# An attention block and two feed-forward layers on one core: the first tile in halves, another order of loads, narrow tiles placed last, one lower part on its own

## The reference

```
scores = cap * tanh(q @ k.T / sqrt(64) / cap)          # 2 batches x 12 heads, 448 tokens, head size 64
attn   = exp(scores - max) / (sum(exp) + 1e-9)
x      = attn @ v                                       # 896 tokens x 768
h      = x @ w_in;  h = max(0.01 * h, h);  y = h @ w_out  # 768 -> 2048 -> 768
yn     = y / rms(y) * rms_g
out    = (silu(yn @ w_gate) * (yn @ w_val)) @ w_out2    # 768 -> 1536 -> 768
```

## Time and profile before

| what | before |
|---|---|
| median of 3 runs | 561.96 us (561.7 to 564.47) |
| the profiled execution's own time | 560.67 us |
| its span, first to last instruction | 558.9 us |
| PE busy | 553.1 us, 99% |
| DVE, POOL, ACT busy | 429.7, 323.6, 290.0 us |

### The profile page before, as it was taken

The page is one execution under the profiler, slowest core; times in us unless marked ns, Lnnn a source line. Parts: engine busy times, 40 slices in busy tenths (PEclk is TensorE's granted clock), DMA queues, the critical chain, the costliest instruction groups (busy, mean ns, idle before and its releaser), DMA issues.

```text
span 558.9 us, 7933 instructions
## 1 busy us (share of the span) xinstructions
PE 553.1 (99%) x2679; PEld 466.1 (83%) x2679; DVE 429.7 (77%) x594; ACT 290.0 (52%) x503; POOL 323.6 (58%) x282
## 2 busy tenths in 40 slices
PE   8999999999999999999999999999999999999997
PEld 5545554699999999999999999999999999999896
DVE  4459988695677799932159498999999999999963
ACT  6888889326445497431155355444434446824330
POOL 1025365478666653594383576766776896634672
PEclk9999999999999999999999999999999999999999
DMA  6254442123111112213022011122211111210521
GB/s 174 70 177 149 135 133 52 37 72 110 62 56 57 57 57 66 86 38 114 1 62 90 0 58 56 58 65 86 77 56 57 57 57 57 62 52 1 154 91 67
DMA packets 30007, 41.49 MB, mean 74 GB/s; under 512 B 17040, under 2 KB 19088, under 8 KB 29968
## 3 DMA queue, kind: packets, MB, share of 16 engines
q1 hardware_dynamic: 29824, 40.99, 23.7%
q10 hardware_dynamic: 144, 0.00, 0.0%
HBM read 38.15 MB, written 2.80 MB: 73 GB/s over the span
## 4 chain that ended last, share of the span: by engine, by line
PE 90%; DVE 6%; issue 2%; DMA 1%; ACT 0%; DVEq 0%; ACTq 0%
PE ps L1763 46%; PE ps L1848 13%; PE ps L1696 9%; PE ps L1933 8%; PE ps L1835 7%; PE ps L1684 3%; PE ps L1702 2%; PE ps L1688 1%; DVE act_lo L1502 1%; DVE x_lo L1502 1%; DMA qk_raw<-in_qk 1%; DVE x_lo_f L1476 1%; DVE act_full L1482 0%; DMA sums<-x_raw 0%; DVE x_raw L1069 0%
## 5 line engine op out<-in xcount | busy, mean ns | idle before, releaser
L644 POOL TENSOR_TENSOR w_lo<-w_raw,w_hi 128x384 fp32r<-128x384 f32 x109 | 128.6, 1189 | 82.3 <-ACT w_hi L757 81.6
L644 POOL TENSOR_TENSOR w_lo<-s_sum,w_hi 128x384 fp32r<-128x384 f32 x112 | 129.6, 1172 | 78.9 <-ACT w_hi L757 78.8
L1763 PE MATMUL ps<-x_hi,w_hi 128*128 128x448 f32 x420 | 154.1, 367 | 0.0
L1763 PE MATMUL ps<-x_hi,w_lo 128*128 128x448 f32 x420 | 153.5, 365 | 0.0
L1763 PE MATMUL ps<-x_lo,w_hi 128*128 128x448 f32 x420 | 153.4, 365 | 0.0
L757 ACT ACTIVATE w_hi<-s_sum 128x384 fp32r<-128x384 f32 x112 | 57.1, 523 | 125.4 <-DVE s_sum L1132 50.1
L1763 PEld LDWEIGHTS ps<-x_hi,w_hi 128*128 128x128 f32 x420 | 78.9, 188 | 7.3 <-issue 0.7
L1763 PEld LDWEIGHTS ps<-x_hi,w_lo 128*128 128x128 f32 x420 | 78.9, 188 | 6.4
L1763 PEld LDWEIGHTS ps<-x_lo,w_hi 128*128 128x128 f32 x420 | 78.9, 188 | 6.2
L757 ACT ACTIVATE w_hi<-w_raw 128x384 fp32r<-128x384 f32 x109 | 55.0, 512 | 20.2 <-PE ps L1835 10.0
L1696 PE MATMUL ps<-probs,v_ones 128*65 128x448 f32 x144 | 56.6, 540 | 0.3 <-DVE x_raw L1069 0.2
(11 more groups left out here) (220 smaller groups left out, 1086.1 us busy)
## 6 DMA issues: line engine op xcount, KB each, us to landing
w_raw<-in_w_out SPq DMA_DIRECT2D x27, 384.0 KB, 3.5
w_raw<-in_w_in SPq DMA_DIRECT2D x16, 384.0 KB, 3.8
qk_raw<-in_qk SPq DMA_DIRECT2D x11, 480.0 KB, 4.5
w_raw<-in_w_gate SPq DMA_DIRECT2D x12, 384.0 KB, 3.0
w_raw<-in_w_val SPq DMA_DIRECT2D x12, 384.0 KB, 3.7
v_ones<-in_v SPq DMA_DIRECT2D x12, 224.0 KB, 3.2
recip_row<-recips SPq DMA_DIRECT2D x12, 224.0 KB, 3.4
out<-sq SPq DMA_DIRECT2D x6, 224.0 KB, 2.0
```

The costliest lines, as they stand in the source:

```text
L644: pool.tensor_tensor(w_lo[:, c], source, w_hi[:, c].bitcast(F32), ALU.subtract).then_inc(w_lo_done, 1)
L1763: last = pe.matmul(ps[:, base(s) + BANK_OF[j], 0:S], w[:, w_c], x[:, xs(j, c)], start=(j in (P1, P5, P7, P6) and c == 0 and w is w_hi and ...
```

## The change

Four things are changed.

1. **The first tile in halves.** The layout of `qk` puts the first 128 keys ahead of the queries. The first load takes these keys and 224 queries (352 columns), the second the other 224 queries, the third the rest. DVE splits them in that order, PE makes the first tile's scores in two halves of the queries (`half_scores`), and ACT does tanh and exp on each half. DVE also makes the third part's upper half, which ACT made before, and takes the reciprocal of `cap` first. Six instead of nine matmuls on zeros stand ahead. PE weighs tile 1 of pair 0 before, not after, the scores (1, 0).
2. **SP's order in the loop over pairs.** `load_qk` of pair 4 stands ahead of the loop, and in the loop `load_qk(p + 5)` stands between `store_recip` and `load_recip_row`. The weight panel stands last.
3. **The narrow tiles** (from `ones` to `rms`) are placed behind `h_sums`, `g` and `spare` instead of ahead of them.
4. **T2's last third.** `z_lo(1, T2, 2)` writes to a place of its own, `z_spare`, and stands ahead of `z_sum(1, T4, 2)`.

```diff
@@ -130,6 +130,13 @@
         sq_acc = buf("sq_acc", B * S, F32)
         sq = [buf(f"sq{s}", S, F32) for s in range(2)]
         ident = buf("ident", 128, F32)
+        RING = place["at"]
+        h_sums = buf("h_sums", 8 * S, F32)
+        G = place["at"]
+        g = buf("g", 2 * N1 * S, F32)
+        SPARE = place["at"]
+        spare = buf("spare", S, F32)
...
@@ -137,11 +144,6 @@
         sums_eps = buf("sums_eps", 2 * S // 128, F32)
         recip = [buf(f"recip{s}", 2 * S // 128, F32) for s in range(2)]
         rms = buf("rms", 3 * 8, F32)
-        RING = place["at"]
-        h_sums = buf("h_sums", 8 * S, F32)
-        G = place["at"]
-        g = buf("g", 2 * N1 * S, F32)
-        spare = buf("spare", S, F32)
...
         at(SQ_ACC)
         z_acc_lo = buf("z_acc_lo", S, F32R)
+        at(SPARE)
+        z_spare = buf("z_spare", S, F32R)
         at(XL)
         x_lo_f32 = buf("x_lo_f32", 7 * KH * S, F32)
...
@@ -269,16 +275,21 @@
         ORDER = (0, 1, MAIN, 2)
-        FIRST = S + 128
+        PART = S // 2
+        FIRST = 128 + PART
+        SECOND = FIRST + PART
         BLOCK_SUMS = {3: [(0, P5)], 5: [(0, P7)], 6: [(0, P6), (0, P3), (1, P5)], 9: [(1, P7)], 10: [(1, P6), (1, P3)]}
-        EXPS = ([(0, 2, 1), (1, 2, 2), (2, 3, 4)], [(0, 4, 2), (2, 3, 4)])
+        HALVES = 2
+        EXPS = ([(1, 2, 2), (2, 3, 4)], [(0, 4, 2), (2, 3, 4)])
         def exps_before(p):
-            return sum(len(EXPS[q > 0]) for q in range(p))
+            return HALVES * (p > 0) + sum(len(EXPS[q > 0]) for q in range(p))
...
             if part == 1 and blk in (B11, B12, B22, B21):
                 return x_lo[:, xs(T1 if blk == B12 else blk, c)]
+            if (part, blk, c) == (1, T2, KH - 1):
+                return z_spare[:, :]
             return z_place(part, blk, c, act_lo, z_acc_lo[:, :], x_lo)
...
             sp.dma_start(qk_raw[0][:, 0:FIRST], qk[0][:, 0:FIRST]).then_inc(first_in, 16)
+            sp.dma_start(qk_raw[0][:, FIRST:SECOND], qk[0][:, FIRST:SECOND]).then_inc(second_in, 16)
...
             load_v(1)
             load_qk(3)
+            load_qk(4)
             for p in range(PAIRS):
                 spread_sums(p)
                 if p + 2 < PAIRS:
                     load_v(p + 2)
-                if p + 4 < PAIRS:
-                    load_qk(p + 4)
+                store_recip(p)
+                if p + 5 < PAIRS:
+                    load_qk(p + 5)
+                load_recip_row(p)
                 if 0 < p < 5:
                     load_raw(p - 1, w_in[p - 1])
-                store_recip(p)
-                load_recip_row(p)
             sp.dma_start(rms_col[:, :], rms_g.rearrange("(c p) -> p c", p=128),
...
+            def first_half():
+                c = tiles(probs_of(0, 0, 2), S)[:, :, 0:PART]
+                act.wait_ge(first_half_scored, 1)
+                act.activation(c, ps[:, bank_of(0, 0):bank_of(0, 0) + 2, 0:PART], ACT.Tanh, scale=capc[:, 4:5]).then_inc(first_half_tanh, 1)
+                act.wait_ge(first_half_tanh, 1)
+                act.wait_ge(consts, 5)
+                act.activation(c, c, ACT.Exp, scale=capc[:, 0:1], bias=capc[:, 6:7]).then_inc(exp_done, 1)
+            def second_half():
+                c = tiles(probs_of(0, 0, 2), S)[:, :, PART:S]
+                act.wait_ge(scores_done, 1)
+                act.activation(c, ps[:, PV:PV + 2, 0:PART], ACT.Tanh, scale=capc[:, 4:5]).then_inc(tanh_done, 1)
+                act.wait_ge(tanh_done, 1)
+                act.activation(c, c, ACT.Exp, scale=capc[:, 0:1], bias=capc[:, 6:7]).then_inc(exp_done, 1)
...
             act.wait_ge(ones_set, 1)
             act.activation(ones[:, 1:2], ones[:, 0:1], ACT.Tanh).then_inc(table_ready, 1)
-            act.wait_ge(qk_in[0], 16)
-            act.activation(qk_hi[0][:, FIRST:QK], qk_raw[0][:, FIRST:QK], ACT.Copy).then_inc(qk_hi_done, 1)
-            act.wait_ge(cap_done, 1)
+            act.wait_ge(consts, 2)
             for p in range(PAIRS):
-                tanh(p, 0)
                 if p == 0:
-                    exp(0, 0)
+                    first_half()
+                    second_half()
+                else:
+                    tanh(p, 0)
                 tanh(p, 1)
                 if p == 1:
                     tanh(1, MAIN)
-                exp(p, int(p == 0))
+                exp(p, 0)
                 if p != 1:
                     tanh(p, MAIN)
                 tanh(p, 2)
-                exp(p, 1 + int(p == 0))
+                exp(p, 1)
                 if 0 <= p - 4 < 7:
                     weight_hi(p - 4)
...
@@ -1181,33 +1214,40 @@
                 dve.wait_ge(prod_done, count[widx(s, P4)])
                 dve.tensor_tensor(g_tile(4 * s + 2), bank(s, BANK_D), u2[s % 2][:, :], ALU.add).then_inc(c21_done, 1)
-            def split_first():
-                c = slice(0, FIRST)
-                dve.wait_ge(first_in, 16)
+            def upper_first(c, landed):
+                dve.wait_ge(landed, 16)
                 dve.tensor_copy(qk_hi[0][:, c], qk_raw[0][:, c]).then_inc(first_hi_done, 1)
-                dve.wait_ge(first_hi_done, 1)
+            def lower_first(k, c):
+                dve.wait_ge(first_hi_done, k + 1)
                 dve.tensor_tensor(qk_lo[0][:, c], qk_raw[0][:, c], qk_hi[0][:, c].bitcast(F32), ALU.subtract).then_inc(first_lo_done, 1)
-            def split_second():
-                c = slice(FIRST, QK)
+            def split_rest():
+                c = slice(SECOND, QK)
+                dve.wait_ge(qk_in[0], 16)
+                dve.tensor_copy(qk_hi[0][:, c], qk_raw[0][:, c]).then_inc(qk_hi_done, 1)
                 dve.wait_ge(qk_hi_done, 1)
                 dve.tensor_tensor(qk_lo[0][:, c], qk_raw[0][:, c], qk_hi[0][:, c].bitcast(F32), ALU.subtract).then_inc(qk_lo_done, 1)
             dve.memset(ones[:, :], 1.0).then_inc(ones_set, 1)
             dve.memset(extra[:, 0:128], 0.0).then_inc(zeros_set, 1)
-            split_first()
+            first_c, second_c = slice(0, FIRST), slice(FIRST, SECOND)
+            upper_first(first_c, first_in)
+            lower_first(0, first_c)
             dve.wait_ge(cap_in, 16)
+            dve.reciprocal(capc[:, 3:4], capc[:, 0:1]).then_inc(consts, 1)
+            dve.wait_ge(consts, 1)
+            dve.tensor_scalar(capc[:, 4:5], capc[:, 3:4], SCALE, None, ALU.mult).then_inc(consts, 1)
+            upper_first(second_c, second_in)
             dve.tensor_scalar(capc[:, 1:2], capc[:, 0:1], -1.0, None, ALU.mult).then_inc(consts, 1)
-            dve.wait_ge(consts, 1)
+            dve.wait_ge(consts, 3)
             dve.tensor_tensor(capc[:, 2:3], capc[:, 0:1], capc[:, 1:2], ALU.max).then_inc(consts, 1)
-            dve.wait_ge(consts, 2)
-            dve.reciprocal(capc[:, 3:4], capc[:, 2:3]).then_inc(consts, 1)
+            dve.wait_ge(consts, 4)
             dve.scalar_tensor_tensor(capc[:, 6:7], capc[:, 2:3], SAFE, capc[:, 2:3], ALU.min, ALU.subtract).then_inc(consts, 1)
-            dve.wait_ge(consts, 4)
-            dve.tensor_scalar(capc[:, 4:5], capc[:, 3:4], SCALE, None, ALU.mult).then_inc(consts, 1)
-            dve.wait_ge(consts, 5)
-            dve.nop().then_inc(cap_done, 1)
-            split_second()
+            lower_first(1, second_c)
+            split_rest()
             split_qk(1)
             for p in range(PAIRS):
...
             def z_lo(part, blk, c):
                 dve.wait_ge(z_hi_done, z_count[part, blk, c])
-                if (part, blk) in ((0, T2), (0, B21), (1, T2)):
+                if (part, blk) in ((0, T2), (0, B21)) or (part, blk) == (1, T2) and c < KH - 1:
                     dve.wait_ge(t4_done[part], c + 1)
                 elif (part, blk) == (1, T3):
                     dve.wait_ge(t2_done[1], c + 1)
@@ -1631,9 +1671,11 @@
             s_part(s + 1, P6, 1)
             z_sums(T2)
             z_lower(1, T3)
-            for c in range(KH):
+            for c in range(KH - 1):
                 z_sum(1, T4, c)
                 z_lo(1, T2, c)
+            z_lo(1, T2, KH - 1)
+            z_sum(1, T4, KH - 1)
             take_p5(s + 1)
             s_part(s + 1, P3, 1)
...
                     if i < MAIN:
                         for h in range(2):
-                            last = pe.matmul(ps[:, bank + h, 0:S], k[HEAD[h], k_c], q[HEAD[h], 0:S],
+                            last = pe.matmul(ps[:, bank + h, 0:S], k[HEAD[h], k_c], q[HEAD[h], q_c],
...
+            def k_cols(i):
+                return slice(0, 128) if i == 0 else slice(S + i * 128, S + (i + 1) * 128)
+            def half_scores(half, bank, scored):
+                hi, lo = qk_hi[0], qk_lo[0]
+                q_c = slice(128 + half * PART, 128 + (half + 1) * PART)
+                pe.wait_ge(first_hi_done, half + 1)
+                for k, q in ((hi, hi), (hi, lo), (lo, hi)):
+                    if q is lo:
+                        pe.wait_ge(first_lo_done, half + 1)
+                    for h in range(2):
```

(19 more changed lines are left out.)

22 lines of the change are left out of this document (10 added, 12 removed).

## The result

The changed kernel takes 566.89 us in the median (563.61 to 568.53, 7 runs) beside 561.70 us of before (560.49 to 564.47, 7 runs): ratio 1.0087, 95% interval 1.0065 to 1.0109. The forecast was 561.0 us, with a range that ended at 563.6 us. The profiled execution took 568.53 us with a span of 566.7 us; of before it was 560.67 and 558.9 us.

The account below looks back on a forecast made before the run. PE was taken as the bound, busy 553.1 of 558.9 us. Panel +1.5, T2 -0.52 and narrow tiles -1.95 gave -0.97 us, from a 561.96 us median to 561.0 us; range 558.9 to 563.6 us.

Parts of the forecast that it names:

- the panel's term: SP's loop of pair 2: panel issued behind the reciprocals' row lands at 43.7 us, 1.5 us later, costing +1.5 us.
- the gains of the other parts: T2's last third -0.52 us and narrow tiles -1.95 us; the start's 0.37 us was taken as swallowed by the panel.
- the 0.07: Chance that the panel is on time and the tiles' address changes nothing: 560.9 us.
- the far bound of +3.7: Panel's latest landing: reciprocals take 2.9 us, panel 5.3 us, landing at 45.9 us, +3.7 us.
- rival 3: Panel's late landing eats all other gains from +2.5 us on; at worst, without the pace gain, 565.1 us; chance 0.05.
- Whatever the start does: Claim that PE at 60.81 us is 18.6 us behind the panel's landing, regardless of any gain at the start.
- the 18.6 us of distance: From the panel's landing before the change to PE at 60.81 us, where it waits 0.16 us for pair 5's copy.
- Rival 4: Start: with six warm-ups the array's clock steps up late, costing 0.5 to 2 us, 561.5 to 563 us; chance 0.08.
- rival 2: Output layers: narrow tiles' address changes nothing, pace follows something else about the stages; 562.9 us; chance 0.25.
- 1.95 us: Gain from narrow tiles placed behind: 1.36 us from 207.6 to 320.2 us, 0.44 in the tail, 0.15 before T2.
- T4's sum is 0.7 us later, and its products come five items later, so nothing waits: Last layer, T2's last third near 517 us: the reordering delays nothing else, so the gain is 0.52 us.
- The forecast of 0.37 us: First tile in halves: PE has its scores at about 8.25 us instead of 8.62 us, gaining 0.37 us.

Follow-up runs that it names:

- the filled wait: Changed kernel with 14 more matmuls on zeros on TensorE ahead of the fifth weighing, where it waits for x_raw: 563.24 us, ratio 1.0038.

## Why the prediction was wrong, by its own steps

The sum was +1.5 for the panel and -2.47 for the other parts. Measured by the ratios, the panel's place was worth 5.1 us in the changed kernel, and what is left without it is -0.2 us. So the failed step is the panel's term, 3.6 us too small, and after it the gains of the other parts, 2.3 us too large. (The chances, with the 0.07 counted by itself, add up to 1.05.)

**The panel.** The mechanism was right, down to the instruction that waits; the term of +1.5 us was mis-sized: it cost 2.7 us with the rest of SP's new order, 3.5 us alone and 5.1 us in the changed kernel, by the ratios. The forecast let the panel leave at 39.7 and land at 43.7 us. It left at 42.99 and landed at 48.37 us. These 4.7 us are: 2.4 by the start (2.04 late instead of 0.37 early), 1.4 by the sums, whose landing had been taken unchanged, 1.4 by the panel's landing (5.4 instead of 4.0), and 0.6 back by the reciprocals (1.4 instead of 2.0). Moved alone, with a start only 0.55 us late, the panel cost 3.5 us; there the reciprocals took 3.1 us and the panel 3.8, and it landed 3.4 us later than before. That is near the far bound of +3.7, the case of rival 3 with its chance of 0.05. Of the chain of three DMAs that wait for each other, the sums were taken as they were, with no range, though before shows landings (min/median/max) of

```profile
DMA to landing us min/median/max: 2.0/2.1/3.4
```

and the other two were given values near the fast end, while the rows of the same place in before showed 4.8 us for the reciprocals and 5.3 us for the panel.

**"Whatever the start does."** This was wrong. The panel is issued behind steps that follow PE, so a late start shifts it too, and the start was not swallowed: in the profiled execution it and the wait add up. Nor was the 18.6 us of distance to the weighing of pair 6 the thing to look at. The copy of `x_raw` stands right behind the waiting instruction, and PE needs it at the very next weighing, for which it was ready near 46.6 us. The forecast named a wait there, of about 1 us; it was 3.6 us.

**The clock, at two places.** Rival 4 (0.08) came true at the start: "by 10.2 us some 2 us"; it was 12.2 us and 2.04 us. The six warm-ups alone make it, without the halves. The fall of the clock in the wait was in no case of the forecast; it was put at nothing without a reason, and it cost about 1.6 us. The Trainium skill ("TensorE: Matmul & The Clock Gate", HAM oscillation — how this bites in real kernels) warns that a wait for a DMA can send the engine back to half rate; the windows above (0.50 behind a wait of 3.6 us) and the filled wait agree.

**The narrow tiles.** The pace of 0.2049 us left the 120-matmul pieces in every version with these tiles behind, so the price was real and rival 2 falls. Of 1.95 us, the runs gave 0.9, 1.1 and 1.6 us by the differences in ratio (alone, in the new order, with the halves). In the traces the output product gives 1.1 us of the 1.36 forecast, and the last layer gives 0.45 us of 0.59 where it runs at the fast pace (79.53 instead of 79.98 us) and loses 0.3 us where it falls into the third pace below (80.26 us).

**T2.** The failed step is "T4's sum is 0.7 us later, and its products come five items later, so nothing waits". T4 does not wait, but `take_p5` is queued behind that sum, and P3 waits for it. Of 0.52 us, 0.2 to 0.3 were left in the profiles and none in the median.

**The halves.** Landing, DVE and ACT were right to 0.1 us. The gain at PE's start was at most 0.46 us, when the clock came in time. The forecast of 0.37 us did not come: on the kernel before, with nine warm-ups, the ratio is 1.0015 (1.0002 to 1.0027), 0.8 us worse; beside the narrow tiles it is 0.2 us worse, within the noise. Whether the halves cost anything stays open. The candidate is the reciprocals' trip of the last pair but one: 2.6 to 2.9 us in all six profiles with a wait for `x_lo`, 1.4 us in eleven of the twelve without, 2.3 us in the changed kernel. Four of the ten profiles with halves have the wait and two of the eight without halves, one of these with no edit at all ahead of the last layer. So chance lengthens the trip too, and one profile of each kernel can't tell whether the halves do.

## What to carry to other kernels

Before a wide load is moved behind a step that waits for another DMA, add up that chain with the slow values of the trace, and look at what is queued behind its consumer and when TensorE needs just that; a long wait can be paid a second time by the clock (here one of 3.6 us was, those of 1.6 to 2.2 us in the profiles were not). Warm-up matmuls are not spare work: with six instead of nine, TensorE stayed slow until after 12 us in three of six profiles here, with either form of the first tile. A step moved ahead of another on a queue needs the whole list of what now stands behind, also the steps that free a bank.

## What the runs showed of the hardware

**The clock.** PE idle for 3.6 us: granted clock 0.50 after it. Idle for 1.6, 2.0 and 2.2 us: the next weighing took 4.70 us in each profile, full clock. But over all runs of these three kernels the mean granted clock was 0.997 in 3 of 8, 3 of 8 and 1 of 6, and it was 0.999 or more in every run of the kernel before, so the clock fell in some of their executions. It was also 0.996 or 0.997 in 7 of 47 runs of the four kernels with six warm-ups and no late panel. At the start of the changed kernel's profile the column of the granted clock reads 1.00 while matmuls take twice their time, so there only durations tell.

**Three paces for one stream.** The same 120 matmuls of 448 columns, with no wait in them, take 24.59 us, 24.32 us (above), and in the changed kernel with nine warm-ups

```profile
298.72 24.80 PE ps L1904 x120
```

that is 0.2049, 0.2027 and 0.2067 us each. The first goes with a streamed tile that starts 32 bytes off a multiple of 64, and vanished in every version with the narrow tiles behind; other offsets were not tried. The third appears with all tiles on such a multiple. It comes in some executions and not in others at the same place (38.09 and 37.37 us for the last 183 matmuls, above), and it lasted from 112 to about 237 us in the changed kernel and from 231 to 339 us with nine warm-ups; what sets it is open. Over the 549 matmuls between 207.6 and 320.2 us in the profile of before it would be worth 2.2 us, as much as most of the effects here, so it is likely to be part of the spread from run to run.
